# Attention, a bilinear layer and four experts on one core: another order of the experts' down and up products inside a block

## The reference

```python
def _attn_ref(q, k, v, alpha):                 # gated linear attention, 4 x 8 heads, 768 steps, 48 wide
    for t in range(S):
        state = alpha[:, :, t, :, None] * state + np.einsum('bhd,bhe->bhde', k[:, :, t], v[:, :, t])
        y[:, :, t] = np.einsum('bhd,bhde->bhe', q[:, :, t], state)

def _moe_ref(x, w1, w2, w3, w_out):            # 3072 tokens, 384 -> 1024 -> 384
    h = (x @ w1) * (x @ w2) @ w3
    return h @ w_out

def _moe2_ref(x, domain_probs, w1, w2):        # 3072 tokens, 4 experts
    p = domain_probs / (domain_probs.sum(-1, keepdims=True) + 1e-09)
    for e in range(E):
        h = np.maximum(x @ w1[e], 0.0)         # up: 384 -> 1024
        out += p[:, e:e + 1] * (h @ w2[e])     # down: 1024 -> 384
```

## Time and profile before

| | before |
|---|---|
| median of three executions | 1224.75 us |
| lowest, highest | 1223.33, 1225.75 us |
| profiled execution | 1223.07 us |
| its span | 1221.3 us |
| TensorE matmul busy | 1216.6 us (100%) |
| TensorE weight load busy | 1113.5 us (91%) |
| VectorE busy | 454.7 us (37%) |
| ScalarE busy | 276.2 us (23%) |
| GpSimd busy | 169.0 us (14%) |
| DMA | mean 88 GB/s |

### The profile page before, as it was taken

How to read it: one execution, slowest core, us unless ns; L and a number is a source line. 1 busy time by engine, 2 the same in 40 slices (tenths; PEclk the granted TensorE clock), 3 DMA queues, 4 the chain that set the end, 5 groups by cost and what they waited for, 6 DMA issues and landing times.

```text
span 1221.3 us, 18784 instructions
## 1 busy us (share of the span) xinstructions
PE 1216.6 (100%) x7714; PEld 1113.5 (91%) x7714; DVE 454.7 (37%) x873; ACT 276.2 (23%) x515; POOL 169.0 (14%) x148
## 2 busy tenths in 40 slices
PE   9999999999999999999999999999999999999998
PEld 5699999999999999999999999999999999999998
DVE  4887686676651122222222222221122222222222
ACT  1443333333333311111111111111111111111111
POOL 1122222222223530000000000000000000000000
PEclk9999999999999999999999999999999999999999
DMA  9624643643514341001141111123001111222201
GB/s 293 214 73 99 163 126 83 165 126 77 156 47 163 121 160 52 23 29 52 53 155 52 52 52 52 52 65 143 27 25 51 52 52 53 78 78 77 78 7 46
DMA packets 84854, 107.49 MB, mean 88 GB/s; under 512 B 36400, under 2 KB 55216, under 8 KB 84272
## 3 DMA queue, kind: packets, MB, share of 16 engines
q1 hardware_dynamic: 84352, 105.91, 27.8%
q10 hardware_dynamic: 432, 0.59, 0.1%
HBM read 86.03 MB, written 18.09 MB: 85 GB/s over the span
## 4 chain that ended last, share of the span: by engine, by line
PE 99%; DVE 0%; issue 0%; DVEq 0%
PE bank L1122 32%; PE bank L1234 25%; PE bank L973 9%; PE score_banks L1234 8%; PE bank L975 8%; PE bank L974 8%; PE bank L1012 2%; PE bank L1168 2%; PE bank L1183 1%; PE score_banks L1033 1%; PE bank L1022 1%; PE score_banks L998 1%; PE bank L1161 0%; PE score_banks L982 0%; DVE total L951 0%
## 5 line engine op out<-in xcount | busy, mean ns | idle before, releaser
L793 DVE SCALAR_TENSOR_TENSOR h_lo<-bank,h_hi 128x512 fp32r<-128x512 f32 x192 | 132.8, 692 | 584.8 <-ACT h_hi L584 583.9
L584 ACT ACTIVATE h_hi<-bank 128x512 fp32r<-128x512 f32 x192 | 114.8, 598 | 661.6 <-PE bank L1122 661.6
L1122 PE MATMUL bank<-x_hi,we_lo 128*128 128x512 f32 x576 | 228.7, 397 | 0.0
L1122 PE MATMUL bank<-x_hi,we_hi 128*128 128x512 f32 x576 | 224.1, 389 | 0.0
L1122 PE MATMUL bank<-x_lo,we_hi 128*128 128x512 f32 x576 | 223.5, 388 | 0.0
L1234 PE MATMUL bank<-we_hi,h_hi 128*128 128x384 f32 x576 | 194.6, 338 | 0.0
L1234 PE MATMUL bank<-we_lo,h_hi 128*128 128x384 f32 x576 | 194.5, 338 | 0.0
L1234 PE MATMUL bank<-we_hi,h_lo 128*128 128x384 f32 x576 | 193.8, 336 | 0.0
L482 POOL TENSOR_TENSOR we_lo<-we_raw,we_hi (+1 forms) x48 | 60.9, 1291 | 527.7 <-ACT we_hi L545 527.5
L1122 PEld LDWEIGHTS bank<-x_hi,we_lo 128*128 128x128 f32 x576 | 108.3, 188 | 22.4
L1122 PEld LDWEIGHTS bank<-x_lo,we_hi 128*128 128x128 f32 x576 | 108.0, 188 | 22.7
(11 more groups left out here) (89 smaller groups left out, 1442.2 us busy)
## 6 DMA issues: line engine op xcount, KB each, us to landing
x_hi<-x_hi_spill SPq DMA_DIRECT2D x24, 768.0 KB, 4.9
x_lo<-x_lo_spill SPq DMA_DIRECT2D x24, 768.0 KB, 6.3
we_raw<-wset SPq DMA_DIRECT2D x4, 3072.0 KB, 10.1
inputs<-akq SPq DMA_DIRECT2D x24, 448.0 KB, 5.2
values<-v_rows SPq DMA_DIRECT2D x24, 256.0 KB, 3.6
inputs<-akq SPq DMA_DIRECT2D x24, 224.0 KB, 3.2
x_hi_spill<-x_hi_out SPq DMA_DIRECT2D x8, 576.0 KB, 4.3
x_lo_spill<-x_lo_out SPq DMA_DIRECT2D x8, 576.0 KB, 5.2
```

Of the source, the lines that this page charges most:

```text
L584: act.activation(h_hi[:, s % 2, :], bank[s % 2][:, :], ACT.Relu).then_inc(h_hi_ready, 1)
L793: dve.scalar_tensor_tensor(out=h_lo[:, s % 2, :], in0=bank[s % 2][:, :], scalar=0.0, in1=h_hi[:, s % 2, :], op0=ALU.max, op1=ALU.subtract) ...
L1122: mm = pe.matmul(bank[s % 2][:, :], (we_hi if term < 2 else we_lo)[e % 2][:, cols], (x1_lo if term == 1 else x1_hi)[u][:, k, :], start=(i ...
```

## The change

In `step2` a block issued its 21 matmuls as three groups of seven: down, down, up, down, up, down, up. Now it issues three down matmuls and then nine pairs of one down and one up.

```diff
--- before.py
+++ after.py
@@ -1241,12 +1241,10 @@
                 pe.wait_ge(h_lo_ready, STEPS2 * (e * ROUNDS + m) + s + 1)
                 if ahead:
                     up2_waits(*ahead)
-                ups = 0
                 for i in range(SUBS * TERMS):
                     down2_product(e, m, s, i)
-                    if ahead and i % SUBS >= 1:
-                        up2_product(ahead[0], ahead[2], ups)
-                        ups += 1
+                    if ahead and i >= TERMS:
+                        up2_product(ahead[0], ahead[2], i - TERMS)
 
             def round2(e, m, following):
 
```

## The result

The changed kernel takes 1231.1 us (four executions, 1230.67 to 1231.66) where the kernel before takes 1224.35 us (four, 1223.33 to 1225.75). The ratio is 1.0057, with a 95% interval from 1.0045 to 1.0069: slower by half a percent, and clear of the scatter between executions. The forecast was slower too, but by 3.3 us, and 1231.1 lies above the range, which ended at 1230.2.

The account below looks back on a forecast made before the run. TensorE's own pace was taken to bound the kernel: 4179 less 6.5 plus 5 gives 4177.5 ns a block, 17.5 over 4160; over 190 blocks 3.3 us, so 1224.75 + 3.3 = 1228.0 us. The range was 1223.0 to 1230.2.

Parts of the forecast that it names:

- the covers: ScalarE's and VectorE's work, bank reuse and a tile's adds stay hidden behind TensorE's matmuls; costed at nothing.
- the plain sum: A block's 12 downs and 9 ups, each at its own kind's price of 173.3 and 233.3 ns: 4179 ns.
- the pairs: The block's nine down-up pairs in steady alternation cost just the two own prices, 406.6 ns each; bounds 0.40 us and 413 ns.
- The rival that finds cheap pairs: In the alternation, pairs go dear and cheap (400 ns) by turns: 5 ns less a block, 1223.8 us; chance 0.10.
- the run of downs adds 5: Third and fourth down at the block's start together cost 5 ns extra, between bounds of 0 and 14.
- full-price rival: Third and fourth down at each block's start cost +14 instead of +5 ns: block 4186.5 ns, 1229.8 us; chance 0.12.
- one meeting of downs a block instead of three leaves one saving of 6.5: Each place in a block where two downs meet saves 6.5 ns; keeping one brings 4179 to 4172.5 ns.
- The order-free rival: Savings depend on a block's number of downs, not their places: block stays 4160 ns, time 1224.75 us; chance 0.28.

Follow-up runs that it names:

- three_two: Same 21 matmuls a block as the kernel before, reordered: three downs, up, four down-up pairs, two downs, up, three pairs; 1226.26 us, ratio 1.0017.
- mid_run: Changed kernel with its three extra downs moved from the block's start to behind the fourth pair; 1231.21 us, ratio 1.0063 to the kernel before.
- runs: Same matmuls as the kernel before, reordered: all 12 downs of a block, then all 9 ups; 1226.54 us, ratio 1.0026.
- fours: Same matmuls as the kernel before, reordered: three times four downs, then three ups; 1232.04 us, ratio 1.0061.
- double_ups: Same matmuls as the kernel before, reordered: three times down, down, up, up, then three times down, down, up; 1224.71 us, ratio 1.001.
- two_ups: Same matmuls as the kernel before, reordered: three times down, down, up, up, down, down, up; 1223.75 us, ratio 1.0001.

## Why the prediction was wrong

**Right: the direction, the bound and the covers.** TensorE's own pace decides; no wait appeared before lines 1234 or 1122. ScalarE and VectorE, the banks and the adds of a tile cost nothing.

**Right: the plain sum and the pairs.** The long alternation costs 174.2 + 232.5 = 406.7 ns a pair; the prediction took 406.6. The rival that finds cheap pairs is out: none of the seven pairs behind the first two is cheap.

**Wrong: "the run of downs adds 5".** This term was the third and the fourth down of a block; the bounds were 0 and 14 ns, from block 191, and I took a third of it, since no row had the fourth down followed by an up. They measured 177.5 and 185: 16 ns over two at 173.3, the full price and a little. The up behind does not soften it. With the first two downs, at 174 and 175, the run is 18 ns over the sum. The full-price rival had this slot right at 0.12.

**Wrong: "one meeting of downs a block instead of three leaves one saving of 6.5".** Among pairs a run of exactly two saved; not each place where downs meet does. There a run of two saves 7, a run of three nothing (three_two), a run of four loses 20 (changed, mid_run). I had read the saving off a row in which every run was two long and extended it to four. The two ups behind the run are at 234 and 233, where the group before has 227 and 226. It is also about half of why even the full-price rival, 4186.5, stayed 13.5 ns a block short of 4200: 6.5 ns are the saving that it kept, and the rest is the run, 20 ns dear with the places around its third and fourth down instead of 14, and the rounding of the sum.

**The sum again**, with the terms as measured: 4180 - 0 + 20 = 4200 against 4180 - 6.5 + 5 = 4178.5 (the text had 4177.5, by a rounded 4179).

**The order-free rival.** The rival in which the price knows no order (the first of the list, which the prediction once calls the second) falls: nine orders of the same matmuls spread over 40 ns a block. The prediction named the Trainium skill beside it (TensorE: Matmul & The Clock Gate, "Back-to-back issue gap"), whose spacing for isolated matmuls has the columns as its only variable; here it is too short, 3892 ns against 4160 to 4200, and neighbours count. That a slot shrinks with the columns, and is not held up by the 188 ns that a weight load shows, is what the 256-column ups have at 113 to 123 ns.

**What stays open.** What carries the history was not found. The experiments exclude, for blocks inside a tile, the place in the block, the evictions and a change of PSUM bank; extra time also comes up without a difference in length. In the changed kernel the slots are the same in every block but the first, over both weight buffers, both input slots and both `h` slots.

That first block says something more. Ahead of it stand nine ups and a wait of TensorE instead of pairs; its own matmuls come in the same order as in every other block:

```profile
423.74 0.44 PE L1234 MATMUL score_banks<-we_hi,h_hi 128*128 128x384 f32 x1
424.02 0.34 PE L1234 MATMUL score_banks<-we_lo,h_hi 128*128 128x384 f32 x1
424.20 0.33 PE L1234 MATMUL score_banks<-we_hi,h_lo 128*128 128x384 f32 x1
424.37 0.33 PE L1234 MATMUL bank<-we_hi,h_hi 128*128 128x384 f32 x1
424.55 0.39 PE L1122 MATMUL bank<-x_hi,we_hi 128*128 128x512 f32 x1
424.77 0.34 PE L1234 MATMUL bank<-we_lo,h_hi 128*128 128x384 f32 x1
```

Behind the first, the slots are 179, 174 and 173, and the up is at 226: no dear fourth down, and a cheap up. In mid_run's first block four pairs stand between that wait and the run, and the run is already at 175, 177, 185. So what makes the run dear lies ahead of it: the same four downs at the same place are cheap behind the nine ups and the wait (which of the two does it is open; in runs nine ups alone did), and four pairs are enough to make them dear. A rule "the price follows from the run's length" is a summary of these orders, not a mechanism: fours has runs of four at +20 and at -7 with the same neighbours, double_ups has six runs of two and saves 13 where two_ups saves 20, and equal widths reorder the ranking. How TensorE hands over from one matmul to the next while the following weights are loaded may be behind it; that is only argued. It could not be tried with fewer weight loads, since each matmul brings its own.

## What to carry to other kernels

When TensorE is busy throughout, the order of matmuls of two kinds can still move the time by half a percent: in this kernel runs of two of the shorter kind among pairs were the cheapest, and a run of four behind strict alternation the dearest. With other widths the ranking was another, so such an order has to be measured for its own widths. Price a reordering with slots (start to start) of a stretch that has the very run lengths, and where a trace holds one rare instance of the new pattern, as block 191 did here, take its price whole. Measure the block, not the kernel: one profile gives its length to about a nanosecond, and so tells orders apart (4.160 and 4.167 us) whose times differ by 0.1%.

## What was unexpected of the hardware

- The same seven matmuls in a repeating pattern settle into two states, 1387 and 1413 ns, that alternate to the end of the kernel (fours).
- Downs can take 168 and 172 ns between double ups (two_ups), while long runs of downs settle at 173.3. What is short in one slot is paid in its neighbours: the seven still take 1387 ns.
- In runs, the ups' slots grow from about 118 ns at 256 columns to 233.3 at 512, so by 0.45 ns a column. That is more than a cycle of the 2.4 GHz level, 0.42 ns, at a granted clock of 1.00.
